# The last 64 tokens of the v projection in two passes with both halves of x side by side, in a fused transformer block on one core

## The reference

```
h = gelu(x @ w_in)                      # 576 x 1024, tanh form of gelu
u, v = h[..., :512], h[..., 512:]
v_n = (v - mean(v)) / sqrt(var(v) + 1e-6) * g_ln     # over the 512 features
v_s = einsum('ts,bsd->btd', w_sg, v_n) + b_sg        # mixes the 576 tokens
x = x + (u * v_s) @ w_out
```

## Time and profile before

| what | value |
|---|---|
| median of 3 runs | 670.52 us (670.43 to 671.32) |
| the profiled execution's own time | 669.66 us |
| its span in the trace | 667.9 us |
| granted TensorE clock, mean | 0.999 of full speed |
| TensorE matmul busy | 654.9 us, 98% of the span |
| VectorE / ScalarE / GpSimd busy | 530.5 / 356.5 / 250.6 us |
| stage A / first matmul of stage B at | 0 to 299.4 us / 299.4 us |

### The profile page before, as it was taken

One profiled execution on the slowest core, in us unless ns is written; L12 is line 12 of the kernel. 1 busy time (PEld: TensorE's weight loads), 2 busy tenths in 40 slices (PEclk: granted clock), 3 DMA queues, 4 the chain that ended last, 5 costly groups with the idle time before them and its releaser, 6 DMA issues. The chain is left out here.

```text
span 667.9 us, 14062 instructions
## 1 busy us (share of the span) xinstructions
PE 654.9 (98%) x5158; PEld 622.4 (93%) x5160; DVE 530.5 (79%) x1162; ACT 356.5 (53%) x897; POOL 250.6 (38%) x258
## 2 busy tenths in 40 slices
PE   8999999999999999999999999999999999999997
PEld 4679998999899998999999999999999999999997
DVE  5967866887779858997885785786999899898883
ACT  7866874488348845335663453354684344444440
POOL 0576331535061528478336456230401512113011
PEclk9999999999999999999999999999999999999999
DMA  8660008000620051128353768859941826517301
GB/s 296 257 240 2 1 3 306 7 2 2 220 110 2 14 188 33 56 80 307 107 170 108 231 233 254 295 188 346 323 150 47 319 78 239 170 50 289 89 19 53
DMA packets 49923, 98.25 MB, mean 147 GB/s; under 512 B 4672, under 2 KB 33216, under 8 KB 47296
## 3 DMA queue, kind: packets, MB, share of 16 engines
q1 hardware_dynamic: 49152, 96.16, 41.7%
q0 software_dynamic: 704, 1.21, 0.8%
HBM read 64.83 MB, written 32.52 MB: 146 GB/s over the span
## 5 line engine op out<-in xcount | busy, mean ns | idle before, releaser
L1886 PE MATMUL pair<-xf_hi,w_hi 128*128 128x288 f32 x896 | 265.8, 297 | 2.9 <-DVE xf_lo L567 1.4
L1887 PE MATMUL pair<-xf_lo,w_hi 128*128 128x288 f32 x896 | 264.3, 295 | 0.0
L1888 PE MATMUL pair<-xf_hi,w_lo 128*128 128x288 f32 x896 | 263.4, 294 | 0.0
L1886 PEld LDWEIGHTS pair<-xf_hi,w_hi 128*128 128x128 f32 x896 | 167.9, 187 | 4.4 <-DVE xf_lo L567 1.9
L1888 PEld LDWEIGHTS pair<-xf_hi,w_lo 128*128 128x128 f32 x896 | 168.7, 188 | 0.0
L1887 PEld LDWEIGHTS pair<-xf_lo,w_hi 128*128 128x128 f32 x896 | 168.1, 188 | 0.0
L1129 ACT ACTIVATE xf_hi<-res 128x576 fp32r<-128x576 f32 x140 | 93.9, 682 | 90.7 <-PE pair L1888 67.7
L1545 DVE TENSOR_TENSOR stage<-pair,stage 128x576 f32<-128x576 f32 x136 | 100.7, 753 | 41.5 <-PE pair L1888 34.6
L567 DVE TENSOR_TENSOR xf_lo<-res,xf_hi 128x576 fp32r<-128x576 f32 x140 | 109.6, 793 | 13.8 <-ACT xf_hi L1129 13.3
L1010 POOL TENSOR_TENSOR xr<-xr,stage 128x576 f32<-128x576 f32 x16 | 33.6, 2102 | 149.4 <-DVE stage L1545 149.3
L1221 ACT ACTIVATE stage<-stage 128x576 f32<-128x576 f32 x64 | 43.6, 683 | 84.6 <-DVE stage L1545 84.6
(11 more groups left out here) (134 smaller groups left out, 1287.8 us busy)
## 6 DMA issues: line engine op xcount, KB each, us to landing
hid_scratch<-stage SPq DMA_DIRECT2D x64, 288.0 KB, 3.2
res<-hid_scratch SPq DMA_DIRECT2D x16, 1152.0 KB, 6.8
w_raw<-w_ff_dram SPq DMA_DIRECT2D x16, 512.0 KB, 4.0
v_sb<-vW_dram SPq DMA_DIRECT2D x16, 384.0 KB, 6.8
xr<-x_scratch SPq DMA_DIRECT2D x16, 288.0 KB, 3.0
out_dram<-xr SPq DMA_DIRECT2D x16, 288.0 KB, 3.2
k_sb<-kT_dram SPq DMA_DIRECT2D x15, 304.0 KB, 6.5
q_sb<-qT_dram SPq DMA_DIRECT2D x15, 288.0 KB, 6.3
```

Source lines behind the costliest of these rows:

```text
L1886: pe.matmul(dst, wh, xh, start=(start and x == 0), stop=False)
L1887: pe.matmul(dst, wh, xl, start=False, stop=False)
L1888: last = pe.matmul(dst, wl, xh, start=False, stop=(stop and x == n - 1))
```

## The change

The last v group multiplies 64 tokens only, so its stationary operand fills half of TensorE's 128 columns. The change places the rounded part and the remainder of these 64 tokens side by side as one stationary operand of 128 columns: one pass with the rounded weights and one with their remainder replace the three passes, in each of the four chunks. The operand is put together by GpSimd (`place_short`) in the memory of `vn_hi[:, 4, :]`, which is free at that time. The result then lies in two halves of the partitions (the product of hi, the product of lo), and they have to be added: ScalarE copies the second half into `gv`, VectorE adds the first half from PSUM, and ScalarE computes gelu in two halves from the sum (`gelu_short`). The product lo·lo is computed too, where it was left out before.

The same edit moves other work. The rounding of the five v tiles goes from VectorE to ScalarE (`round_v`), one tile behind each of the first five u groups. The fifth split goes from GpSimd to VectorE (`split_last_v`). In batches 1 and 2 the second half of the squares moves behind the copy of the last v group on ScalarE, their sum moves from VectorE to GpSimd, and the copy of the first variance on ScalarE moves ahead of the exponentials. The diff, cut to its core:

```diff
+        xop = sb("xop", [P, 2, KC, S], F32R, phase_a)
+        xop_hi, xop_lo = xop[:, 0, :, :], xop[:, 1, :, :]
...
+        xshort = vn_hi[:, NS - 1, :].rearrange("p (k i t) -> p k i t", k=KC, i=2)
...  # GpSimd
+            def place_short(b, pair):
+                pool.wait_ge(x_lo, b * PAIRS + (pair + 1))
+                if b >= 1:
+                    pool.wait_ge(group_ready, (b - 1) * len(GROUPS) + NGELU + NMIX)
+                pool.tensor_copy(xshort[:, pair, :, :],
+                                 xop[:, :, pair, S - LAST:S]).then_inc(x_short, 1)
...
                 for s in range(NS):
                     if s + 1 < NS:
                         root_v(b, s + 1)
-                    split_v(b, s)
+                        split_v(b, s)
...
                 split_all_v(b)
+                if b >= 1:
+                    sum_chunks(pool, 4 * (b - 1) + 3)
...
+                    for pair in {4: (0, 1), 6: (2,), 7: (3,)}.get(t, ()):
+                        place_short(b + 1, pair)
...  # ScalarE
             def gelu_v(b, s):
...
+                act.activation(gv[0:LAST, s, :], bank[GROUP_BANK[s]][LAST:P, :], ACT.Copy).then_inc(short_copied, 1)
+
+            def gelu_short(b):
+                s = NS - 1
+                act.wait_ge(short_added, b + 1)
+                act.activation(gv[LAST:P, s, :], gv[0:LAST, s, :], ACT.Gelu_apprx_tanh).then_inc(short_doubled, 1)
+                act.wait_ge(short_doubled, b + 1)
+                act.activation(gv[0:LAST, s, :], gv[0:LAST, s, :], ACT.Gelu_apprx_tanh).then_inc(gelu_done, 1)
+
+            def round_v(b, s):
+                act.wait_ge(vn_done, b * NS + (s + 1))
+                act.activation(vn_hi[:, s, :], gv[:, s, :], ACT.Copy).then_inc(vnh_ready, 1)
...
                 if norm and not last:
-                    for h in range(2):
-                        squares(n, h)
+                    squares(n, 0)
                 for s in range(NS):
                     gelu_v(b, s)
+                    if norm and not last and s == NS - 1:
+                        squares(n, 1)
...
+                gelu_short(b)
                 for g in range(NS, NGELU):
                     gelu_u(b, g)
+                    if g < 2 * NS:
+                        round_v(b, g - NS)
...  # VectorE
+            def add_short(b):
+                x = gv[0:LAST, NS - 1, :]
+                dve.wait_ge(short_copied, b + 1)
+                dve.tensor_tensor(x, bank[GROUP_BANK[NS - 1]][0:LAST, :], x, ALU.add).then_inc(short_added, 1)
+
             def v_norm(b, s):
...
-                dve.wait_ge(vn_done, b * NS + (s + 1))
-                dve.tensor_copy(vn_hi[:, s, :], gv[:, s, :]).then_inc(vnh_ready, 1)
+
+            def split_last_v(b):
+                dve.wait_ge(vnh_ready, (b + 1) * NS)
+                dve.tensor_tensor(vn_lo[:, NS - 1, :], gv[:, NS - 1, :], vn_hi[:, NS - 1, :].bitcast(F32),
+                                  ALU.subtract).then_inc(vnl_ready, 1)
...
                     if s >= 1:
                         v_norm(b, s - 1)
+                    if s == 1:
+                        add_short(b)
...
+                if b in (1, 2):
+                    split_sum(dve, 4 * (b - 1) + 2)
+                split_last_v(b)
...
-                if norm:
-                    split_sum(dve, 4 * n + 2)
-                    sum_chunks(dve, 4 * n + 3)
...  # TensorE
-                    pe.wait_ge(x_lo, b * PAIRS + (k + 1))
+                    pe.wait_ge(x_short if s == NS - 1 else x_lo, b * PAIRS + (k + 1))
+                    if s == NS - 1:
+                        for w in (win_hi, win_lo):
+                            last = pe.matmul(bank[GROUP_BANK[s]], vn_hi[:, NS - 1, k * P:(k + 1) * P], w[:, k, GATE:],
+                                             start=(k == 0 and w is win_hi), stop=(k == KC - 1 and w is win_lo))
+                        continue
```

More of the change, by code:

```diff
@@ L206, in sequence_block_kernel @@
         win_lo = sb("win_lo", [P, KC, 2 * GATE], F32R, phase_a)
-        xop_hi = sb("xop_hi", [P, KC, S], F32R, phase_a)
-        xop_lo = sb("xop_lo", [P, KC, S], F32R, phase_a)
+        xop = sb("xop", [P, 2, KC, S], F32R, phase_a)
+        xop_hi, xop_lo = xop[:, 0, :, :], xop[:, 1, :, :]
         wsg_hi = sb("wsg_hi", [P, NS, S], F32R, phase_a)
@@ L312, in sequence_block_kernel @@
         x_act, x_dve = sem("x_act"), sem("x_dve")
-        x_hi, x_lo = sem("x_hi"), sem("x_lo")
+        x_hi, x_lo, x_short = sem("x_hi"), sem("x_lo"), sem("x_short")
         group_ready = sem("group_ready")
         gelu_done = sem("gelu_done")
+        short_copied, short_added, short_doubled = sem("short_copied"), sem("short_added"), sem("short_doubled")
         bn_done, aggr_done = sem("bn_done"), sem("aggr_done")
@@ L845, in split_x @@
                                    ALU.subtract).then_inc(x_lo, 1)
+                if b == 0:
+                    place_short(b, pair)
+            def place_short(b, pair):
[4 more added lines that the diff above has]
+                                 xop[:, :, pair, S - LAST:S]).then_inc(x_short, 1)
             def root_v(b, s):
@@ L966, in _ @@
             split_x(0, 2)
-            pool.wait_ge(x_lo, PAIRS)
+            place_short(0, PAIRS - 1)
             for c in range(1, KC):
@@ L1060, in gelu_v @@
             def gelu_v(b, s):
+                if s < NS - 1:
+                    act.wait_ge(group_ready, b * len(GROUPS) + (s + 1))
+                    act.activation(gv[:, s, :], bank[GROUP_BANK[s]], ACT.Gelu_apprx_tanh).then_inc(gelu_done, 1)
+                    return
                 act.wait_ge(group_ready, b * len(GROUPS) + (s + 1))
-                for rows in (slice(0, P),) if s < NS - 1 else (slice(0, LAST), slice(LAST, P)):
-                    last = act.activation(gv[rows, s, :], bank[GROUP_BANK[s]][0:rows.stop - rows.start, :],
-                                          ACT.Gelu_apprx_tanh)
-                last.then_inc(gelu_done, 1)
+                act.activation(gv[0:LAST, s, :], bank[GROUP_BANK[s]][LAST:P, :], ACT.Copy).then_inc(short_copied, 1)
[8 more added lines that the diff above has]
+                act.activation(vn_hi[:, s, :], gv[:, s, :], ACT.Copy).then_inc(vnh_ready, 1)
             def gelu_u(b, g):
@@ L1170, in period @@
                         copy_pT(b + 1, 2 * t - 2)
+                    if b >= 1 and t == 0:
+                        copy_variance(b - 1, 0)
                     if t < QUADS:
@@ L1184, in period @@
                         round_gated(b, 2 * t)
-                    if b >= 1 and t == 0:
-                        copy_variance(b - 1, 0)
             def last_period(b):
```

## The result

The changed kernel takes 675.35 us (median of 6 runs, 674.41 to 677.64) against 670.47 us (6 runs, 669.87 to 671.60): the ratio is 1.0071, with a 95% interval of 1.0057 to 1.0085. It is slower, by 3.8 to 5.7 us, inside the range of 668.4 to 676.0, with 673.9 forecast. The profiled execution took 677.43 us (span 675.6), one of two of the six above 677.

A forecast was written before the change was run, and what follows sets the result against it. TensorE, busy 98%, bounds the kernel, with 0.6 us slack on the chain feeding it. Losses of 1.25 + 0.33 + 0.33 + 1.5 = 3.4 us on 669.66 give 673.06, plus 0.86 for the median: 673.9, range 668.4 to 676.0.

The forecast's parts named there:

- The saving: TensorE's last v group: eight matmuls instead of twelve, 0.23 us each, save 0.92 us a batch, 3.68 in four.
- The chain of batches 1 and 2: Steps from the last v group to the first mix product: mix 1.25 us later, less 0.92, 0.33 lost per batch.
- E': Start of a batch's first u product, also the end of its last v group, after the change.
- the step of GpSimd: One split and root on GpSimd, taken as 2.43 us, setting the time from split 0 to split 3.
- Batch 3: Mix at E' + 14.3, net 0.5 us later, and TensorE waiting 1.0 at the out groups: 1.5 lost.
- Batch 0: First mix product waits for VectorE's last w_sg split: 2.15 us later, less 0.92, 1.25 lost.
- The port order: Batch 0: GpSimd's first w_out split gets the shared ports before VectorE's w_sg split; otherwise only 0.2 us is lost.
- a rival that did not happen: The start of the attention hit too, 676.5 us, chance 0.15; the range to 676.0 leaves out half of it.
- VectorE gets the ports first: Rival: norm 4 issued ahead of split 3 takes 0.55 us instead of 1.50; 669.1 us, chance 0.18 with far end.
- This is the wait that the change adds.: GpSimd's roots 2 to 4 queue behind split 0, which waits for ScalarE's rounding until E' + 4.2; norms wait for roots.
- Only base loss: Rival: batch 0 loses 0.2 us, batch 3 makes up VectorE's delay and loses 0.5; 671.9 us, chance 0.15.
- the attention is hit: Rival: late exponentials make transposes wait, up to 1.28 us more in batches 1 and 2; 676.5 us, chance 0.15.

The follow-up runs named there:

- e9: Changed kernel with all v splits on VectorE, batch 0's last w_sg split behind norm 3, and three passes again in the last v group; ratio 1.0013 to before.
- e6: Changed kernel with each GpSimd split s held until VectorE's norm s + 1 is done; ratio 1.0129 to the kernel before.
- e2: Changed kernel with GpSimd's roots 2 and 3 ahead of split 0 and root 4 behind it; ratio 0.9982 to the kernel before.
- e3: Kernel before with the two-pass last v group alone, none of the moves of other work; ratio 1.0006 to the kernel before.
- e5: Changed kernel with GpSimd's four v splits on VectorE too, GpSimd keeping only the roots there; ratio 0.9947 to the kernel before.
- e7: e2 with VectorE's last w_sg split in batch 0 one norm earlier, behind norm 3; ratio 0.9944 to the kernel before.
- e8: e5 with VectorE's last w_sg split in batch 0 one norm earlier, behind norm 3; ratio 0.9933 to the kernel before.
- e4: Changed kernel with the last v group in three passes again, all moves of other work kept; ratio 1.0038 to the kernel before.
- e10: Changed kernel with the rounding of the v tiles back on VectorE, behind each norm; ratio 1.0056 to the kernel before.
- e11: Changed kernel with both halves of the squares ahead of the gelus again in batches 1 and 2; ratio 1.0107 to the kernel before.
- e1: Changed kernel run once more, with nothing altered; ratio 1.0064 to the kernel before.

## Why the prediction was right

**The saving.** Predicted 0.23 us a matmul and 0.92 a batch: measured 1.82 us for eight, and 3.70 for all (e9).

**The chain of batches 1 and 2.** Predicted split 0 at E' + 4.2, split 3 at 11.5, the end of norm 4 at 13.0, the statistic at 14.8, mix at 15.5. Measured in batch 2: 4.48, 11.35, 12.92, 14.76, 15.45. Two errors of the sum cancel in this. Its own terms for ScalarE add up to 4.3 (0.8 + 1.35 is 2.15 and not 2.05, and the last two steps add 0.96 and not 0.90), and split 0 came 0.28 late; the step of GpSimd was 2.29 us and not 2.43, which took back 0.4 in three steps. The loss at the mix is 0.30 us, 0.33 was predicted. Not in the sum: batch 2 got 0.35 us back behind the mix, since a transpose no longer waits 0.43 us for the variance, and batch 1 lost 0.1 there.

**Batch 3.** Predicted mix at E' + 14.3 and 1.0 lost at the out groups, 1.5 in all. Measured: E' + 14.04 and 1.15, 1.4 in all. The wait came at the very product that the prediction named (296.21 before, 300.23 now), which lost 0.8; small hold-ups at the out products ahead of it make the rest.

**Batch 0, a term too small.** Predicted 1.25 us lost, measured 1.83 (16.60 - 13.85 - 0.92). Norm 4 was to end at E' + 12.9 and ended at 13.34 (56.96 + 1.50): split 0 came 0.24 late, and the three steps to split 3 took 7.49 us and not 7.3, as roots 3 and 4 took 0.93 us (the row at 55.99) and not the 0.72 of the earlier trace rows. All that follows is late by 0.5, and the mix starts 0.11 us behind the end of the last split, which the sum did not have. The w_sg split of tile 3, which the prediction does not have in this place, costs nothing: it ends at 59.13, as the rounding does that the last v split needs. The port order was forecast rightly: GpSimd's w_out split went first (59.73), and the last w_sg split took 1.73 us beside it and ended at 61.61.

**What cancelled, and what was luck.** Stage A lost 3.53 us against 3.4 forecast, but batch 0 lost 0.6 more than its term and batches 1 to 3 together 0.4 less. The time itself, 675.35, lies 0.15 above the forecast's own range of 672.3 to 675.2. It is inside the stated range because that reaches up to a rival that did not happen.

**The clock, not in the sum at all.** A wait of 2.7 us in batch 0 lets TensorE's clock fall in about half of the executions. Over the changed kernel's 14 runs, 7 have a mean granted clock of 0.997 or less, and their median is 675.8 us; that of the other 7 is 674.5. So of the 1.45 us between the forecast of 673.9 and the 675.35, stage A's chain is 0.1 and the clock, at 1.5 us in half of the runs, about 0.75 (an estimate). The other 0.6 are not told apart from the scatter of stage B.

**The rival "VectorE gets the ports first".** It didn't come about in the changed kernel, and as a mechanism it was wrong: I counted the 0.95 us that the norm wins and not what each split behind a norm loses (0.66 us of waiting, e6). Its worth is on the other side.

**"This is the wait that the change adds."** That was right, and e2 shows it: with the roots ahead of the splits the waits at the statistic and the mix groups of batches 1 to 3 are gone. That with the moves the second statistic of batches 1 and 2 comes 0.4 us late once the chain is hidden was not in the prediction (it is not a part of the 3.53: there the waits ahead of it are longer). The sixteen copies, put at nothing, cost 0.1 us. "Only base loss" and "the attention is hit" did not happen.

## What to carry to other kernels

A strictly ordered engine passes one late input on to everything behind it: look at what stands behind an instruction that will now wait, and put the short steps of the chain (here the roots) ahead of it; the same instructions in another order made 4.8 us of loss into a gain of 1.2, and with one more reorder a gain of 3.8. A saving on the busiest engine is worth what the slack of the chain that feeds it leaves over, and here a few tenths were left: the saving without the better order gained nothing (e3), nor did the better order without the saving (e9). Where two engines share ports, ask whose idle time the lock uses up before it is fought.

## What the runs showed of the hardware

TensorE's clock can fall to half behind a single wait, and whether it does varies from execution to execution. In batch 0 the waits, and the runs with a mean granted clock of 0.997 or less: no wait or 0.2 us (before, e3, e5, e7 to e9) 9 of 92; 1.2 and 1.6 us (e4, e2) 1 of 18; 2.7 us (changed kernel) 7 of 14; 3.4 and 4.2 us (e10, e6) 10 of 10; and e11, with 2.7 us in batch 0 and 1.9 in batch 2, 3 of 4. The mean clock is only a sign of a fall: it doesn't say where it was, and the 9 of 92 show how often it is that low without such a wait. In the profiles, the granted clock behind the wait went down to 0.50 to 0.52 in e1, e6, e10 and e11, and stayed at 1.00 in the first profile of the changed kernel. In e6 the stretch from 64 to 66 us is at 0.50:

```profile
core 0: us, PE busy (x) PEld busy (x) DVE busy (x) ACT busy (x) POOL busy (x), PEclk, DMA share, GB/s
60.00:62.00 2.00, 0.00 (x0) 0.00 (x0) 1.97 (x2) 2.00 (x6) 2.00 (x2) 1.00 0.01 4
62.00:64.00 2.00, 0.73 (x5) 0.76 (x6) 1.97 (x8) 1.98 (x3) 2.00 (x2) 0.93 0.00 0
64.00:66.00 2.00, 2.00 (x10) 2.00 (x10) 1.22 (x12) 1.99 (x12) 2.00 (x3) 0.50 0.05 12
```

Each fall costs 1.4 to 1.5 us, since the mix matmuls run at steps of 0.24 instead of 0.13 us for some 3 us. In e11 it also fell behind a wait of 1.86 us, ahead of which only a few small products of the attention had run (busy 0.20 of the two microseconds from 204 to 206). That idleness halves the clock is what the Trainium skill says too (TensorE: Matmul & The Clock Gate, section "Part 1: The HAM clock gate"); in these runs one wait of 2.7 us did it in 7 of 14 executions.
